# Three stages in one kernel: rounding queries and keys a step sooner, spreading GpSimd's adds, moving a column fold and a row copy

## The chip, the cores and the metric

The kernel runs on one core of one Trainium2 chip. Its time is the device time of one execution in microseconds (us), lower is better; the median of several runs is given.

## The reference, cut to what matters

All numbers are float32. Inputs of the attention are q, k, v of 4 batches x 8 heads x 576 tokens x 64.

```python
def phi(x):                                   # per head, w_phi 64 x 128
    proj = x @ w_phi
    proj = proj - max(abs(proj), axis=-1)
    return concat(exp(proj), exp(-proj))
kv = phi(k).T @ v; z = phi(k).sum(tokens)
x = (phi(q) @ kv) / (phi(q) @ z + 1e-6)       # 4 x 576 x 512 with the heads side by side
u = x + real(fft(fft(x, axis=tokens), axis=features))
un = (u - mean(u)) / sqrt(var(u) + 1e-6)
x2 = u + relu(un @ w_ch1) @ w_ch2             # hidden 2048: the first channel MLP
u2 = x2 + (relu(x2.T @ w_tok1) @ w_tok2).T    # token MLP
out = u2 + relu(u2 @ w_ch1b) @ w_ch2b         # hidden 1536: the second channel MLP
```

## The kernel before, in words

Every large product is made in three passes: each operand is rounded to a high part (ScalarE, `fp32r`), the rest is a low part (a subtraction on VectorE or GpSimd), and TensorE adds hi x hi, hi x lo and lo x hi. So each product needs a rounding and a split first.

The five engines (SP queues DMAs, TensorE, ScalarE, VectorE, GpSimd) each run one hand-written order of instructions, with waits on semaphores. An instruction that waits holds back everything behind it in its engine's order. The change touches the first stage (`front`) and its seam to the first channel MLP.

**The pair loop.** Attention goes through 16 pairs of heads, four pairs to a batch. Step k (from -1 to 15) has five sub-steps s = 0 to 4. In it TensorE projects pair k + 1 in five units (`pe_project`, L273 to L275: a rest of 64 tokens, two key units KA and KB, two query units QA and QB), turns the queries of pair k (`pe_turn`, L284, L288), makes `kv` (L302) and `num` (L316). VectorE's `dve_shift` reads each projected unit: absolute row maximum (L589), then subtraction (L597, `pm`). There are two projection banks, so a unit can be projected when the one two places before has been subtracted. ScalarE takes the exponentials (`ek` L449, `eq` L463). At s = 2 of step k VectorE normalises pair k - 1 (`dve_norm`, L602, L604, L611) into `x_all`.

**Queries and keys.** SP loads them (`load`, L220, L221) with the values (L226). ScalarE rounds them (`act_round`, L436): keys of pair k + 2 at s = 2, queries at s = 4. GpSimd splits them (`pool_split`, L716) at the start of a step: `pool_step(k)` does pair k + 2. `qk` has two buffers by parity of the pair.

**The transform.** Its symmetries halve it. For each pair's 128 columns VectorE adds the two token halves (`dve_sum`, L622, into `fold_s`) and GpSimd subtracts them (`pool_fold`, L728, into `fold_d`). Behind the third and fourth pair of a batch the columns are folded too: `dve_even` (L628) on `fold_s`, and L735 to L738 on `fold_d` and `edge`. ScalarE rounds the folded tables (`act_fold`, L483), VectorE takes the low parts (`dve_low`, L635). TensorE then does 11 pieces per batch (`pe_piece`: five "s" pieces over tokens, L322 to L325, then a cosine and a sine piece for each of three row tiles), two banks in turn. ScalarE copies (L493, L498, L501) and VectorE subtracts (`ab_lo` L644; `less`, `more` L652, L653). The pieces of batch b run one to a sub-step in steps 4b + 5 to 4b + 7. GpSimd adds the results into `x_all` (`pool_add`, four instructions L747 to L751 for each of three row tiles) and finishes token 288 (`pool_row`, L757, L758), which needs `row288`, a copy that ScalarE takes before the first add (`act_row`, L473) into one buffer, free when the row of the batch before is done (`row_done`).

The order of GpSimd's step before:

```python
        if k == PAIRS - 1:
            mlp1["gpsimd"](pool, (), 0, 2)
        for n in ready(k):
            pool_fold(pool, Pair(n))
        if k % 4 == 3 and b >= 0:
            pool_add(pool, b, 0)
            if k < PAIRS - 1:
                pool_add(pool, b, 1)
        if k % 4 == 0 and b >= 1:
            pool_add(pool, b - 1, 2)
            pool_row(pool, b - 1)
```

**The seam.** The 11 pieces of the last batch (`LAST` = 3) run inside the first block of the first channel MLP. That block has 16 hidden chunks j: `pe_first` (L983 to L985, chunk j + 2) and `pe_second` (L997 to L999, chunk j) take turns. `tensor_beside`, `scalar_beside` and `vector_beside` insert the transform's work after a chunk. ScalarE rounds the weights of a chunk (`act_weights`, L1172), GpSimd splits them (L945); `pe_first` of chunk j waits for split j + 1. At step 15 VectorE also does the normalisation of block 0 (`early_norm`: L1064 to L1071, four small steps of 1/sqrt, then L1078 three times), behind which TensorE turns the normed rows (L968). In ScalarE's order `act_row` of the last batch stands behind chunk 0 and ahead of the activation of chunk 1 (L1029); it waits for `row_done` of batch 2. GpSimd does weight chunks 2 and 3 ahead of the last two adds and the row of batch 2.

The three stages behind (first channel MLP from its second block on, token MLP, second channel MLP) are not touched.

## Time and profile before

| what | value |
|---|---|
| median of 3 runs | 1038.95 us (1037.57 to 1039.57) |
| the profiled execution | 1037.23 us, its span 1035.4 us |
| TensorE busy (PE) | 1011.9 us, 98% of the span, 7731 instructions |
| weight loads (PEld) | 905.3 us, 87% |
| VectorE / ScalarE / GpSimd busy | 391.8 us (38%) / 290.4 us (28%) / 188.1 us (18%) |
| chain that ended last | PE 91%; DVE 4%; POOL 3%; ACT 1%; issue 1% |
| mean granted TensorE clock | 0.992 of full |
| L436 rounding of queries or keys (ScalarE) | 32, median 0.67 us |
| L716 their split (GpSimd) | 32, mean 1.44 us |
| L589, L597 on VectorE | 0.69 us each for a full unit, 0.42 for the rest |
| ScalarE waits for turned queries (L463 <- L288) | 43.6 us in 22 waits |
| loads of queries or keys, issue to landing | 4.0 us median, 288 KB each |

Busy times are shares of the span from the first to the last instruction. A matmul's end is modelled, so a busy TensorE is not one at its peak. The front takes about the first 257 us; from there on TensorE hardly waits. PE, DVE, ACT, POOL and SP are TensorE, VectorE, ScalarE, GpSimd and the DMA queue of the Sync engine. In a timeline row the first number is the start, the second the duration, both in us; a bracket gives the idle time of the engine ahead of it and what ended it. The granted clock is given as a share of 2.4 GHz.

### The profile page before, as it was taken

The numbers are of one execution on the slowest core, as the hardware profiler recorded it, in microseconds if no ns is written. First come the engines' busy times: TensorE is split into PE (matmuls) and PEld (weight loads), VectorE is DVE, ScalarE is ACT, GpSimd is POOL, SyncE is SP. The second block draws the span as 40 slices with busy tenths as digits, with TensorE's granted clock in tenths as the row PEclk, the third lists the DMA queues.
The fourth block names the chain that finished last, engine by engine and source line by source line (L and its number), as shares of the span: only waits on it lengthen the run. The fifth ranks groups of instructions, "written<-read, shape, count | busy, mean of one in ns | idle before, by whom it ended". The sixth has DMA issues, their size and how long they took to land.

```text
span 1035.4 us, 18136 instructions
## 1 busy us (share of the span) xinstructions
PE 1011.9 (98%) x7731; PEld 905.3 (87%) x7731; DVE 391.8 (38%) x690; ACT 290.4 (28%) x580; POOL 188.1 (18%) x159
## 2 busy tenths in 40 slices
PE   7999999997999999999999999999999999999998
PEld 5999898986999999999999999777889899999997
DVE  5697878882142231222222213545121212121211
ACT  5765555652331111111111113243111111111110
POOL 2552735474930000000000000053100000000000
PEclk9999999998999999999999999999999999999999
DMA  5322232332601001010010120576101010101000
GB/s 174 97 81 66 73 119 73 132 134 66 191 18 62 1 31 31 1 61 0 0 61 0 48 52 1 168 242 225 46 1 61 1 62 1 61 0 61 0 32 30
DMA packets 47649, 66.34 MB, mean 64 GB/s; under 512 B 22432, under 2 KB 23392, under 8 KB 47456
## 3 DMA queue, kind: packets, MB, share of 16 engines
q1 hardware_dynamic: 45856, 59.10, 18.2%
q10 hardware_dynamic: 1728, 6.29, 1.7%
q8 instruction: 51, 0.84, 0.3%
q14 instruction: 14, 0.11, 0.0%
HBM read 46.51 MB, written 18.87 MB: 63 GB/s over the span
## 4 chain that ended last, share of the span: by engine, by line
PE 91%; DVE 4%; POOL 3%; ACT 1%; issue 1%; DMA 0%; SPq 0%; DVEq 0%; ACTq 0%; POOLq 0%
PE mlp_y L998 11%; PE mlp_y L999 11%; PE mlp_hid L985 11%; PE mlp_hid L983 11%; PE mlp_hid L984 11%; PE mlp_y L997 11%; PE num L316 3%; PE kv L302 3%; PE proj L273 2%; PE four L322 1%; PE proj L274 1%; PE proj L275 1%; PE mlp_turn_in L968 1%; PE four L325 1%; PE tok_y L1262 1%; PE four L324 1%
## 5 line engine op out<-in xcount | busy, mean ns | idle before, releaser
L1097 DVE SCALAR_TENSOR_TENSOR mlp_h_lo<-mlp_hid,mlp_h_hi 128x384 fp32r<-128x384 f32 x168 | 93.7, 558 | 468.6 <-ACT mlp_h_hi L1029 468.6
L983 PE MATMUL mlp_hid<-mlp_ut_hi,mlp_w_hi 128*128 128x384 f32 x672 | 229.2, 341 | 0.0
L985 PE MATMUL mlp_hid<-mlp_ut_hi,mlp_w_lo 128*128 128x384 f32 x672 | 226.5, 337 | 0.0
L984 PE MATMUL mlp_hid<-mlp_ut_lo,mlp_w_hi 128*128 128x384 f32 x672 | 225.5, 336 | 0.0
L1029 ACT ACTIVATE mlp_h_hi<-mlp_hid 128x384 fp32r<-128x384 f32 x168 | 82.6, 492 | 501.1 <-PE mlp_hid L985 501.1
L999 PE MATMUL mlp_y<-mlp_w_hi,mlp_h_lo 128*128 128x512 f32 x504 | 199.6, 396 | 0.0
L998 PE MATMUL mlp_y<-mlp_w_lo,mlp_h_hi 128*128 128x512 f32 x504 | 199.1, 395 | 0.0
L997 PE MATMUL mlp_y<-mlp_w_hi,mlp_h_hi 128*128 128x512 f32 x504 | 197.6, 392 | 0.4 <-DVE mlp_h_lo L1097 0.2
L945 POOL TENSOR_TENSOR mlp_w_lo<-mlp_w_raw,mlp_w_hi 128x1024 fp32r<-128x1024 f32 x26 | 62.5, 2421 | 409.8 <-DVE tok_x_lo L1317 396.5
L983 PEld LDWEIGHTS mlp_hid<-mlp_ut_hi,mlp_w_hi 128*128 128x128 f32 x672 | 126.3, 188 | 5.7 <-DVE mlp_ut_lo L1083 0.2
L984 PEld LDWEIGHTS mlp_hid<-mlp_ut_lo,mlp_w_hi 128*128 128x128 f32 x672 | 126.3, 188 | 5.3
L985 PEld LDWEIGHTS mlp_hid<-mlp_ut_hi,mlp_w_lo 128*128 128x128 f32 x672 | 126.0, 188 | 0.0
L999 PEld LDWEIGHTS mlp_y<-mlp_w_hi,mlp_h_lo 128*128 128x128 f32 x504 | 94.6, 188 | 20.4
L997 PEld LDWEIGHTS mlp_y<-mlp_w_hi,mlp_h_hi 128*128 128x128 f32 x504 | 95.0, 188 | 16.0 <-issue 0.5
L998 PEld LDWEIGHTS mlp_y<-mlp_w_lo,mlp_h_hi 128*128 128x128 f32 x504 | 94.8, 188 | 16.0
L589 DVE TENSOR_REDUCE absmax<-proj 128x4 f32<-128x512 f32 (+1 forms) x80 | 50.5, 632 | 35.3 <-PE proj L275 35.1
L716 POOL TENSOR_TENSOR qk_lo<-qk,qk_hi 128x576 fp32r<-128x576 f32 x32 | 46.1, 1444 | 96.6 <-ACT qk_hi L436 96.6
L273 PE MATMUL proj<-wphi_hi,qk_hi 128*128 128x256 f32 x144 | 48.7, 338 | 10.1 <-DVE pm L597 6.2
L463 ACT ACTIVATE eq<-pt 128x512 f32<-128x512 f32 (+1 forms) x96 | 42.0, 490 | 50.1 <-PE pt L288 43.6
L597 DVE TENSOR_TENSOR pm<-proj,absmax 128x512 f32<-128x512 f32 (+1 forms) x80 | 51.1, 638 | 5.1 <-ACT ek L449 0.5
L1083 DVE TENSOR_TENSOR mlp_ut_lo<-mlp_turn_in,mlp_ut_hi 128x384 fp32r<-128x384 f32 x44 | 24.5, 558 | 73.6 <-ACT mlp_ut_hi L1022 73.4
L449 ACT ACTIVATE ek<-pm 128x512 f32<-128x512 f32 (+1 forms) x96 | 48.4, 558 | 4.4 <-DVE pm L597 4.4
(123 smaller groups left out, 1166.4 us busy)
## 6 DMA issues: line engine op xcount, KB each, us to landing
mlp_u<-u_scratch SPq DMA_DIRECT2D x12, 768.0 KB, 4.6
mlp_w_raw<-in_w_mlp SPq DMA_DIRECT2D x14, 512.0 KB, 4.4
mlp_w_raw<-in_w_mlp ACTq DMA_DIRECT2D x12, 512.0 KB, 7.1
v<-in_v SPq DMA_DIRECT2D x16, 320.0 KB, 3.7
qk<-in_kT SPq DMA_DIRECT2D x16, 288.0 KB, 4.0
qk<-in_qT SPq DMA_DIRECT2D x16, 288.0 KB, 4.0
u_scratch<-x_all SPq DMA_DIRECT2D x4, 1152.0 KB, 6.6
x_scratch<-mlp_u SPq DMA_DIRECT2D x5, 768.0 KB, 3.6
```

Of the source, the lines that this page charges most:

```text
L273: nc.tensor.matmul(out, hi, wphi_hi[:, :], start=True, stop=False)
L589: nc.vector.tensor_reduce(absmax[:, unit, 0:cols], src, AX.X, ALU.max, apply_absolute_value=True).then_inc(absmax_done, 1)
L597: nc.vector.tensor_tensor(pm[p.parity][:, unit, 0:cols, :], src, top, ALU.subtract).then_inc(shifted, 1)
L945: nc.gpsimd.tensor_tensor(w_lo[:, nf - 1 - j, :], raw(j), w_hi[:, j, :], ALU.subtract).then_inc(w_split, 1)
L983: nc.tensor.matmul(out, w_hi[:, j, col], hi, start=(c == 0), stop=False)
L984: nc.tensor.matmul(out, w_hi[:, j, col], lo, start=False, stop=False)
L985: last = nc.tensor.matmul(out, w_lo[:, nf - 1 - j, col], hi, start=False, stop=(c == DC - 1))
L997: nc.tensor.matmul(y[t][:, :], hi, w_hi[:, j, D:2 * D], start=(j == 0), stop=False)
L998: nc.tensor.matmul(y[t][:, :], hi, w_lo[:, nf - 1 - j, D:2 * D], start=False, stop=False)
L999: last = nc.tensor.matmul(y[t][:, :], lo, w_hi[:, j, D:2 * D], start=False, stop=(j == nf - 1))
L1029: nc.scalar.activation(h_hi[:, j % 2, :], hid[j % 2][:, 0:BT], ACT.Relu).then_inc(h_rounded, 1)
L1097: nc.vector.scalar_tensor_tensor(out=h_lo[:, j % 2, :], in0=hid[j % 2][:, 0:BT], scalar=0.0, in1=h_hi[:, j % 2, :], op0=ALU.max, op1=ALU.s ...
```

## The change

Four things are moved; no arithmetic is added or left out.

- Queries and keys of pair k + 3 are both rounded at s = 4 of step k (before: keys of pair k + 2 at s = 2, queries at s = 4). `load` is split into `load_qk` and `load_v`, and the queries and keys of pair n + 1 are loaded ahead of the values of pair n. `pool_split` stays at its place.
- `pool_add` 0, 1 and 2 of a batch stand at the start of three steps (k % 4 = 3, 0, 1), ahead of `pool_fold`; `pool_row` follows the third. `pool_fold` waits for VectorE's sum of the pair, not for its normalisation.
- `dve_even` moves from s = 2 to the end of s = 4 of its step, behind the last two shifts.
- At the seam all five "s" pieces of the last batch stand behind chunk 0, the six others behind chunk 1. ScalarE's `act_row` moves behind the five pieces and behind the activation of chunk 1, and its folds come ahead of weight chunk 2. GpSimd does the last two adds and the row of batch 2 ahead of weight chunks 2 and 3. SP stores batch 2 before it loads weight chunk 6.

```diff
@@ -214,11 +214,13 @@
         return four[(len(PIECES) * b + i) % 2]
 
 
-    def load(sp, p):
+    def load_qk(sp, p):
         if p.n >= 2:
             sp.wait_ge(qk_split, 2 * p.n - 2)
         sp.dma_start(qk[:, p.parity, KEY], dram["kT"][p.n]).then_inc(k_loaded[p.parity], 16)
         sp.dma_start(qk[:, p.parity, QUERY], dram["qT"][p.n]).then_inc(q_loaded[p.parity], 16)
+
+    def load_v(sp, p):
         if p.n >= 2:
             sp.wait_ge(kv_done, p.n - 1)
         else:
@@ -233,11 +235,16 @@
     def sync(sp):
         sp.dma_start(wphi[:, :], dram["wphi"]).then_inc(consts_loaded, 16)
         sp.dma_start(ident_a[:, :], dram["ident"]).then_inc(consts_loaded, 16)
-        load(sp, Pair(0))
-        load(sp, Pair(1))
+        load_qk(sp, Pair(0))
+        load_v(sp, Pair(0))
+        load_qk(sp, Pair(1))
+        load_v(sp, Pair(1))
         sp.dma_start(table[:, 0:TCOLS], dram["table"]).then_inc(table_loaded, 16)
+        load_qk(sp, Pair(2))
         for n in range(2, PAIRS):
-            load(sp, Pair(n))
+            if n + 1 < PAIRS:
+                load_qk(sp, Pair(n + 1))
+            load_v(sp, Pair(n))
             if n in (11, 15):
                 store(sp, n // 4 - 2)
         sp.wait_ge(qk_split, 2 * PAIRS)
@@ -250,9 +257,9 @@
         mlp1["load_weights"](sp, 0, [2, 3])
         sp.wait_ge(x_done, PAIRS)
         mlp1["load_block"](sp, 1)
-        mlp1["load_weights"](sp, 4, [0, 1, 2])
+        mlp1["load_weights"](sp, 4, [0, 1])
         store(sp, 2)
-        mlp1["load_weights"](sp, 4, [3])
+        mlp1["load_weights"](sp, 4, [2, 3])
         mlp1["load_weights"](sp, 8, [0, 1, 2])
         store(sp, 3)
         mlp1["load_weights"](sp, 8, [3])
@@ -425,7 +432,7 @@
 
     def tensor_beside(pe, what, j):
 
-        for i in {("second", 0): (0, 1), ("first", 2): (2, 3), ("second", 1): range(4, len(PIECES))}.get((what, j), ()):
+        for i in {("second", 0): range(5), ("second", 1): range(5, len(PIECES))}.get((what, j), ()):
             pe_piece(pe, LAST, i)
 
 
@@ -517,8 +524,8 @@
                     act_qexp(act, p, 1)
                 if following < PAIRS:
                     act_kexp(act, Pair(following), KA)
-                if k + 2 < PAIRS:
-                    act_round(act, Pair(k + 2), KEY)
+                if k < 0:
+                    act_round(act, Pair(1), KEY)
             if s == 3:
                 if k >= 0:
                     act_kv(act, p)
@@ -526,8 +533,11 @@
                 if following < PAIRS:
                     act_kexp(act, Pair(following), KB)
             if s == 4:
-                if k + 2 < PAIRS:
-                    act_round(act, Pair(k + 2), QUERY)
+                if k < 0:
+                    act_round(act, Pair(1), QUERY)
+                if k + 3 < PAIRS:
+                    act_round(act, Pair(k + 3), KEY)
+                    act_round(act, Pair(k + 3), QUERY)
                 if k % 4 == 1 and 5 <= k:
                     act_fold(act, k // 4 - 1, 1)
                 if k % 4 == 2 and 6 <= k:
@@ -561,18 +571,17 @@
     def scalar_beside(act, j):
 
         if j == 0:
-            mlp1["act_weights"](act, [2])
             act_fold(act, LAST, 0)
             act_fold(act, LAST, 1)
-            mlp1["act_weights"](act, [3])
+            mlp1["act_weights"](act, [2, 3])
+        if j == 1:
+            for i in range(5):
+                act_piece(act, LAST, i)
             act_row(act, LAST)
-        if j == 1:
-            act_piece(act, LAST, 0)
-            act_piece(act, LAST, 1)
             act.wait_ge(fold_split, 2 * B)
             mlp1["act_weights"](act, [4])
         if j == 2:
-            for i in range(2, len(PIECES)):
+            for i in range(5, len(PIECES)):
                 act_piece(act, LAST, i)
             mlp1["act_weights"](act, [5])
         if j == 3:
@@ -665,8 +674,8 @@
                 dve_norm(dve, Pair(k - 1))
                 for n in [0, 1, 2] if k == 3 else [k - 1] if k > 3 else []:
                     dve_sum(dve, Pair(n))
-                    if n % 4 >= 2:
-                        dve_even(dve, n // 4, n % 4 - 2)
+            if s == 4 and k >= 3 and (k - 1) % 4 >= 2:
+                dve_even(dve, (k - 1) // 4, (k - 1) % 4 - 2)
             if s == 4 and k % 4 == 1 and 5 <= k:
                 dve_low(dve, k // 4 - 1, 1)
             if s == 4 and k == PAIRS - 2:
@@ -700,10 +709,10 @@
             dve_low(dve, LAST, 0)
             dve_low(dve, LAST, 1)
         if j == 1:
-            dve_piece(dve, LAST, 0)
-            dve_piece(dve, LAST, 1)
+            for i in range(5):
+                dve_piece(dve, LAST, i)
         if j == 2:
-            for i in range(2, len(PIECES)):
+            for i in range(5, len(PIECES)):
                 dve_piece(dve, LAST, i)
         if j == 9:
             dve.wait_ge(row_done, B)
@@ -719,7 +728,7 @@
     def pool_fold(pool, p):
         b, i = p.n // 4, p.n % 4
         cols = slice(2 * DH * i, 2 * DH * i + 2 * DH)
-        pool.wait_ge(x_done, p.n + 1)
+        pool.wait_ge(summed, p.n + 1)
         if b > 0:
             pool.wait_ge(fold_split, 2 * b)
         else:
@@ -765,27 +774,27 @@
             pool.wait_ge(table_rounded, k + 1)
             nc.gpsimd.tensor_tensor(table_lo[:, THIRD[k]], table[:, THIRD[k]], table_hi[:, THIRD[k]],
                                     ALU.subtract).then_inc(table_split, 1)
+        if k % 4 == 3 and b >= 0:
+            pool_add(pool, b, 0)
+        if k % 4 == 0 and b >= 1:
+            pool_add(pool, b - 1, 1)
+        if k % 4 == 1 and b >= 1:
+            pool_add(pool, b - 1, 2)
+            pool_row(pool, b - 1)
         if k == PAIRS - 1:
             mlp1["gpsimd"](pool, (), 0, 2)
         for n in ready(k):
             pool_fold(pool, Pair(n))
-        if k % 4 == 3 and b >= 0:
-            pool_add(pool, b, 0)
-            if k < PAIRS - 1:
-                pool_add(pool, b, 1)
-        if k % 4 == 0 and b >= 1:
-            pool_add(pool, b - 1, 2)
-            pool_row(pool, b - 1)
 
     def gpsimd(pool):
         pool_split(pool, Pair(0))
         for k in range(-1, PAIRS):
             pool_step(pool, k)
         pool_fold(pool, Pair(PAIRS - 1))
-        mlp1["gpsimd"](pool, (), 2, 4)
         pool_add(pool, LAST - 1, 1)
         pool_add(pool, LAST - 1, 2)
         pool_row(pool, LAST - 1)
+        mlp1["gpsimd"](pool, (), 2, 4)
         pool_add(pool, LAST, 0)
         pool.wait_ge(d_done, 2 * FRONT * B)
         mlp1["gpsimd"](pool, (), 4, 6)
```

## Rows read from the trace of the kernel before

**Rows 1.** TensorE's waits, whole span: us in total, times, longest us.
```profile
PE four L322 <- DVE ab_lo L644: 6.8, 1, 6.8
...
PE proj L273 <- DVE pm L597: 6.2, 8, 2.2
```

**Rows 2.** Busy time by stretch: PE, PEld, DVE, ACT, POOL, clock, DMA, GB/s.
```profile
120.00:130.00 10.00, 7.77 (x133) 7.25 (x131) 8.81 (x11) 4.00 (x9) 9.71 (x13) 0.83 0.30 87
...
240.00:250.00 10.00, 7.47 (x30) 5.96 (x31) 2.75 (x6) 3.69 (x8) 0.43 (x1) 0.58 0.59 170
```

**Rows 3.** TensorE's timeline, num products of a pair: start us, us, what.
```profile
67.00 3.02 PE L316 MATMUL num<-kvs,eq 128*64 128x65 f32 x96
...
78.52 3.02 PE L316 MATMUL num<-kvs,eq 128*64 128x65 f32 x96
...
119.80 3.02 PE L316 MATMUL num<-kvs,eq 128*64 128x65 f32 x96
...
135.07 3.02 PE L316 MATMUL num<-kvs,eq 128*64 128x65 f32 x96
...
176.33 3.02 PE L316 MATMUL num<-kvs,eq 128*64 128x65 f32 x96
...
190.55 3.02 PE L316 MATMUL num<-kvs,eq 128*64 128x65 f32 x96
...
218.89 3.02 PE L316 MATMUL num<-kvs,eq 128*64 128x65 f32 x96
```

**Rows 4.** Timeline 117 to 123.5 us, VectorE and GpSimd.
```profile
118.43 2.09 DVE L622 TENSOR_TENSOR table<-x_all 96x384 f32<-96x384 f32 x1
...
120.56 3.03 DVE L628 TENSOR_TENSOR table<-table 96x384 f32<-96x384 f32 x1
...
119.48 0.62 POOL L751 TENSOR_TENSOR x_all<-x_all,less 96x255 f32<-96x255 f32 x1
...
120.07 3.10 POOL L716 TENSOR_TENSOR qk_lo<-qk,qk_hi 128x576 fp32r<-128x576 f32 x2
```

**Rows 5.** Source line L628: duration ns min/median/max, first, last start.
```profile
L628 DVE TENSOR_TENSOR table<-table x8: 551/1776/3029, 57.2 to 225.1; 96x381 f32<-96x381 f32 x4, 96x384 f32<-96x384 f32 x4
```

**Rows 6.** Timeline around 111 us, VectorE and GpSimd.
```profile
110.83 0.41 DVE L653 TENSOR_TENSOR more<-even,four 96x258 f32<-96x258 f32 x1
...
110.99 1.41 POOL L716 TENSOR_TENSOR qk_lo<-qk,qk_hi 128x576 fp32r<-128x576 f32 x1 [3.46 <-ACT qk_hi L436]
```

**Rows 7.** Timeline around 211 us and 294 us, VectorE and GpSimd.
```profile
211.00 0.41 DVE L653 TENSOR_TENSOR more<-even,four 96x258 f32<-96x258 f32 x1
...
211.53 0.16 DVE L1066 TENSOR_TENSOR mlp_step<-mlp_rstd 128x3 f32<-128x3 f32 x1
...
211.73 0.16 DVE L1068 SCALAR_TENSOR_TENSOR mlp_step<-mlp_step,mlp_var_eps 128x3 f32<-128x3 f32 x1
...
294.17 2.38 POOL L945 TENSOR_TENSOR mlp_w_lo<-mlp_w_raw,mlp_w_hi 128x1024 fp32r<-128x1024 f32 x1 [1.80 <-ACT mlp_w_hi L1172]
...
294.26 2.32 DVE L1071 SCALAR_TENSOR_TENSOR mlp_rstd<-mlp_step,mlp_rstd 128x3 f32<-128x3 f32 x1
```

**Rows 8.** Timeline 223 to 259 us, VectorE, GpSimd, ScalarE, TensorE.
```profile
223.99 0.74 DVE L622 TENSOR_TENSOR table<-x_all 96x384 f32<-96x384 f32 x1
...
228.35 5.54 DVE L635 TENSOR_TENSOR fold_lo<-table,fold_hi 97x774 fp32r<-97x774 f32 x2 [1.19 <-ACT fold_hi L483]
...
227.59 5.48 POOL L945 TENSOR_TENSOR mlp_w_lo<-mlp_w_raw,mlp_w_hi 128x1024 fp32r<-128x1024 f32 x2
...
240.52 0.62 ACT L473 COPY row<-x_all 1x512 f32<-1x512 f32 x1 [10.59 <-POOL x_all L758]
...
249.66 0.30 PE L322 MATMUL four<-table_hi,fold_hi 96*128 96x288 f32 x1
...
256.88 0.34 PE L983 MATMUL mlp_hid<-mlp_ut_hi,mlp_w_hi 128*128 128x384 f32 x1
...
258.96 0.39 PE L997 MATMUL mlp_y<-mlp_w_hi,mlp_h_hi 128*128 128x512 f32 x1
```

## The prediction

> **What bounds the kernel now.** I read the page first: TensorE is busy 98% of the span (first line of the table above), so time can only be gained where it stands still, runs at the lower clock, or waits inside matmuls. The list of waits names two such places: 6.8 us once, before a product of the transform, released by VectorE's low part, and 6.2 us in 8 pieces before projections, released by the subtraction of the row maximum (pm) [rows 1]. The table of stretches adds the clock: 0.83 in 120 to 130 us, 0.58 in 240 to 250 us [rows 2]. I then took TensorE's timeline and used the start of the 96 "num" products as a clock for the pair loop [rows 3]. From pair 4 to pair 5 it takes 78.52 - 67.00 = 11.52 us with no wait in it. The same work takes 135.07 - 119.80 = 15.27 us from pair 8 to 9 and 190.55 - 176.33 = 14.22 us from pair 12 to 13. So 3.75 and 2.70 us are lost there. Both have the same wait of 2.2 us; only the first falls to the lower clock, so a fall costs about 1.05 us. Behind pair 3 there is a small loss of the same kind.
>
> Who makes VectorE late there: the row sum (L622) takes 2.09 us and the column fold (L628) 3.03 us [rows 4], against 0.55 us at best for the fold, and for the sum of the same size [rows 5]. GpSimd is working through four adds and two splits just then. The fold ends 0.5 us after the second split. VectorE's operation with two operands in SBUF stands until GpSimd's run ends. It is let in between the last add and the split (118.43 + 2.09 = 120.52, GpSimd's add ended 120.10), but not between the four adds, nor between the two splits.
>
> The large wait is at the end: ScalarE waits 10.59 us to copy row 288 of the last batch [rows 8], because GpSimd does two weight chunks before the adds and the row of batch 2. Everything behind the copy in ScalarE's order, then VectorE, then TensorE, is late.
>
> **The change, part by part.**
>
> (1) *Pairs 8 and 12.* GpSimd's adds are spread and `pool_fold` waits for the row sum, so GpSimd is idle when that sum comes: 0.55 us in place of 2.09. The fold leaves its place ahead of the last two key and query shifts. Together they take 5.1 - 0.55 = 4.6 us out from in front of a wait of 2.2 us. What is late next is the fold itself, which now stands ahead of the next pair's first shift. It is requested about 121.75 (sum done at 119.0, then two shifts of two operations of 0.69), while GpSimd is in the last instruction of its fold; then come two splits. Let in at that border, it costs nothing and the whole 3.75 and 2.70 come back. If it is let in only behind both splits (two of 1.4 us), TensorE waits 1.9 us. I take 3.75 and 2.70, as the border add to split is of this kind; lower ends 1.9 and 0.8.
>
> (2) *Pairs 7 and 11.* The fold of batch 1 (and 2) used to hide ahead of shifts that were early. It now follows VectorE's "more", which ends at 111.24 and can come up to 0.4 us earlier, while GpSimd starts its split at 110.99 [rows 6]. If VectorE is first, nothing is lost; if not, it waits for both splits (2.8 us) and the next first shift, for which I estimate 1.6 us of room in TensorE's timeline, comes 1.2 us late. I take 0.4 each, ends 0 and 1.2. *Pair 3:* three sums now compete with three GpSimd folds that start behind each sum; gain 0.4 to loss 1.1, taken as 0.
>
> (3) *Queries and keys a step sooner.* 32 roundings and 32 splits stay, as do all DMAs. No pair but the first two was late by them, so I cost the move at nothing. Cover: ScalarE waits 43.6 us in 22 waits for the turned queries, most of it right behind the new place, and both roundings are 1.3 us (table above). On SP the loads of pair n + 1 stand ahead of the values of pair n; both are needed a step later and a load lands in 4.0 us. If that cover were gone, each pair would pay the 1.3 us. On ScalarE the second rounding of `fold_hi` comes 0.65 us later at pairs 5, 9, 13, where GpSimd is no longer in VectorE's way: 0.
>
> (4) *Pair 15: a new collision.* The first add of batch 2 now comes ahead of the weight chunks, and is released by the same "more" (211.00 + 0.41) that VectorE follows with the four small steps of 1/sqrt (0.2 us apart, [rows 7]). These have operands in SBUF. That such a tiny one is blocked is shown further on: L1071 took 2.32 us and ended with GpSimd's 2.38 us chunk [rows 7]. So L1068 waits for the four adds (to about 214.4), L1071 for the first weight chunk (to 216.9), and the normed rows, 213.6 before, come at 218.6. Behind them on VectorE are "less/more", the normalisation of pair 14 and its row sum. The normalisation ends at 220.8, and the num products of pair 15, which started at 218.89 [rows 3], wait for it: 1.95 us lost. If GpSimd is also ahead of L1066, which starts 0.12 us after "more", one turn more is lost: 4.5 us. The two starts are too close to tell; I take the middle, 3.3.
>
> The Trainium skill, "SBUF — State Buffer", section "SBUF: two separate sides", says that the port pair of GpSimd and VectorE is locked for one whole instruction and then given up. By that rule L1068 would wait for one add of 0.7 us only and this part would cost nothing. The trace shows 2.09 us behind four adds, so I do not follow it here.
>
> (5) *The end of the front.* Count from the start of num 15 (before 218.89) to the fourth hidden chunk (before 256.88): 38.0 us [rows 3, 8]. Now ScalarE's copy stands behind five pieces, and GpSimd does adds and row before chunks 2 and 3. The bound becomes GpSimd. Row sum 15 ended 5.8 us behind num 15 (223.99 + 0.74), and with the column fold of batch 2 now ahead of it comes at 6.3. GpSimd's fold takes 3.3 us, with VectorE's last column fold let in, 3.85; then one low part of VectorE (0.9), an add of 2.75 (four instructions of 0.6 to 0.7), the other low part (0.9), an add (2.75), the row (two of 0.7) and weight chunk 2 (2.4). Sum 21.25. Then TensorE: chunk 2, 2.1 (258.96 - 256.88), its y product 2.1, and six pieces, 6.1 (seven took 256.88 - 249.66 = 7.2). Sum 31.55, gain 6.5. If VectorE's low part is not let in ahead of the first add, 2.8 less: 3.7. (The low parts: two in 5.54 us, of which about 3.7 are waits for the chunks.) If chunk 2 is not what TensorE waits for, its own work and the two conversions give 8.3. Two stalls of about 2 us remain, each of a size at which the clock fell once and once not: 1.05 each at risk, taken as 0.
>
> Sum: 3.75 + 2.70 - 0.8 - 3.3 + 6.5 = 8.9 us. The profiled execution took 1037.23 us (span 1035.4); less 8.9 is 1028.3. The median of the runs is 1.7 above the profiled one, so I forecast **1030.0 us**.
>
> **The rivals.**
>
> *A. VectorE is let in at every instruction of GpSimd.* Then (2) and (4) cost nothing: 3.75 + 2.7 + 6.5 = 13 us, 1026.0. This is the skill's rule above ("SBUF — State Buffer"). For it: the low part L635 got in between the two weight chunks [rows 8]. Against: the four adds and the pair of splits [rows 4]. Chance 0.15.
>
> *B. Late turns eat half.* The folds are let in only behind the splits (pairs 8, 12: 2.7 us returned in place of 6.45; pairs 7, 11: 1.2 lost each) and the rest as in the sum: 2.7 - 2.4 - 3.3 + 6.5 = 3.5 us, 1035.5. For it: the fold's 3.03 us went past the border of two splits. Against: it needs GpSimd to win four near races. Chance 0.22.
>
> *C. Slower: the 1/sqrt chain at pair 15.* It loses three turns (4.5 us) and its late normalisation puts the last sum, fold and low parts of batch 3 behind GpSimd's adds, so that the tail gives only 3.7; with the clock fallen at the waits (two of 1.05) and B's turns lost (2.7 - 2.4): 0.3 - 4.5 + 3.7 - 2.1 = -2.6, so 1041.6. It decides once the chain ends after about 219. For it: the collision is certain, only its length is open. Against: all turns must be lost. Chance 0.07.
>
> *D. No difference.* B with three turns lost in the chain: 3.5 - 1.2 - 1.05 (clock) = 1.2 us, 1037.7. Chance 0.08.
>
> **How the numbers follow.** The forecast, with its own range of 1027 to 1033.5, has 0.48; A 0.15, B 0.22, D 0.08, C 0.07. The range leaves out C, D and the far half of A: 1025.5 to 1036.8. About 0.2% (2.1 us) is what a measurement of this kernel can tell from no change. Faster 0.84 (forecast, A, nearly all of B), same 0.09, slower 0.07.
>
> **What the profile of the changed kernel would show.** (1) right: num 8 to 9 and num 12 to 13 take 11.5 to 12 us, L622 there 0.55; wrong if 13 or more. (2): L628 at pairs 7 and 11 takes 0.55 (VectorE first) or 3 us. (4) right: L1068 and L1071 take 2 to 3 us each, and num 13 to num 15 takes 30.3 to 32.8 us in place of 218.89 - 190.55 = 28.3 [rows 3]; wrong if they take 0.16. (5) right: ScalarE's wait for row 288 is gone and TensorE's longest wait in the tail is about 2 us, for the third weight chunk, after 31 to 32 us. The forecast falls if a wait for a query or key shows up on TensorE or if ScalarE's roundings stand in front of an exponential that TensorE waits for.

## The result, and the profile after

The changed kernel takes 1035.8 us (median of 20 runs, 1034.1 to 1038.4), the kernel before beside it on the same chip 1037.95 us (20 runs): ratio 0.9982, interval 0.9974 to 0.9989. That is faster by 2.15 us. 8.9 us were forecast. The time lies inside the range, at its upper end, but three quarters of the gain are missing.

The profiled execution took 1037.61 us (span 1035.8), which is 1.8 above the median of its own runs, so its span says nothing of a gain. A second profile of the same kernel took 1035.41 us (span 1033.6). I therefore read distances between fixed marks, with both profiles side by side. The first view is TensorE's timeline of the changed kernel, the starts of the num products of pairs 4, 8, 9, 12, 13, 14 and 15. They answer to [rows 3]; pair 4 and 14 are new.

```profile
72.22 3.02 PE L323 MATMUL num<-kvs,eq 128*64 128x65 f32 x96
...
124.99 3.02 PE L323 MATMUL num<-kvs,eq 128*64 128x65 f32 x96
...
137.95 3.02 PE L323 MATMUL num<-kvs,eq 128*64 128x65 f32 x96
...
179.21 3.02 PE L323 MATMUL num<-kvs,eq 128*64 128x65 f32 x96
...
192.18 3.02 PE L323 MATMUL num<-kvs,eq 128*64 128x65 f32 x96
...
208.28 3.02 PE L323 MATMUL num<-kvs,eq 128*64 128x65 f32 x96
...
223.68 4.25 PE L323 MATMUL num<-kvs,eq 128*64 128x65 f32 x96 [0.36 <-DVE x_all L620]
```

In the same view num 3 starts at 56.29. Worked out from such starts (us; "tail" is from num 15 to the fourth hidden chunk, "undisturbed" what the same step takes with nothing late; the other kernels of this study have their numbers with them):

| kernel | num 3 to 4 | 8 to 9 | 12 to 13 | 14 to 15 | tail |
|---|---|---|---|---|---|
| before | 11.18 | 15.27 | 14.22 | 12.23 | 37.99 |
| after, first profile | 15.93 | 12.96 | 12.97 | 15.40 | 33.56 |
| after, second profile | 17.18 | 12.98 | 12.98 | 15.40 | 31.15 |
| undisturbed | 11.2 | 11.5 | 11.5 | 12.2 | |

So against the kernel before the first profile has +4.75, -2.31, -1.25, +3.17 and -4.43, and the first num product starts 0.57 later (its key came later by 0.5): sum +0.5, and the span grew by 0.4. The second has +6.00, -2.29, -1.24, +3.17, -6.84 and an earlier start by 0.50: sum -1.7, and the span shrank by 1.8. No other step moved by more than about 0.1 us.

TensorE's list of waits over the whole span of the changed kernel (first profile):

```profile
PE proj L280 <- DVE pm L606: 7.5, 6, 3.8
PE proj L280 <- POOL qk_lo L725: 5.2, 2, 2.7
PE mlp_hid L992 <- POOL mlp_w_lo L954: 2.6, 1, 2.6
PE mlp_turn_in L977 <- DVE mlp_un L1087: 2.4, 1, 2.4
```

The wait of 6.8 us of [rows 1] is gone. In its place stand 2.6 us for a weight chunk and 2.4 us for the normed rows, and the wait for pm is larger than before (7.5 us against 6.2), with one piece of 3.8 us. The 5.2 us for the splits are at the start, where the loads arrive.

**Pair 3** is the largest loss, and has the piece of 3.8 us. The timeline of VectorE, GpSimd and TensorE from 55 to 67 us:

```profile
55.23 2.30 DVE L631 TENSOR_TENSOR table<-x_all 96x384 f32<-96x384 f32 x3
...
60.10 3.98 DVE L637 TENSOR_TENSOR table<-table 96x381 f32<-96x381 f32 x1
...
59.97 0.99 POOL L747 TENSOR_TENSOR table<-table 96x381 f32<-96x381 f32 x1
60.92 2.75 POOL L725 TENSOR_TENSOR qk_lo<-qk,qk_hi 128x576 fp32r<-128x576 f32 x2
...
65.00 0.39 PE L280 MATMUL proj<-wphi_hi,qk_hi 128*128 128x256 f32 x1 [3.78 <-DVE pm L606]
```

The column fold starts four VectorE operations behind the sums, when GpSimd has one instruction of its own fold and two splits in a row to do. It is let in when the second split ends (63.67) and takes 3.98 us for work of 0.55. Behind the wait the granted clock falls, from 60 to 70 us (columns as in [rows 2]; a slice's clock is its mean, and 0.83 or 0.67 is a slice in part at 2.4 GHz and in part at 1.2 GHz). In the second profile it is 0.66 there behind the same wait of 3.8 us, which goes with the difference between 15.9 and 17.2:

```profile
60.00:70.00 10.00, 6.22 (x91) 5.51 (x91) 9.22 (x12) 3.93 (x8) 4.03 (x4) 0.83 0.01 2
...
240.00:250.00 10.00, 7.41 (x29) 6.82 (x29) 1.54 (x4) 2.74 (x5) 6.23 (x5) 0.67 0.68 219
```

**Pair 8**, the same two engines at 123.6 to 130 us (the lines that answer to [rows 4]):

```profile
123.61 0.55 DVE L631 TENSOR_TENSOR table<-x_all 96x384 f32<-96x384 f32 x1
...
126.81 3.34 DVE L637 TENSOR_TENSOR table<-table 96x384 f32<-96x384 f32 x1
...
125.98 1.00 POOL L747 TENSOR_TENSOR table<-table 96x384 f32<-96x384 f32 x1
126.95 2.79 POOL L725 TENSOR_TENSOR qk_lo<-qk,qk_hi 128x576 fp32r<-128x576 f32 x2
```

The sum is down to 0.55 us as forecast, the fold is not: 3.34 us instead of 3.03, in a later place.

**Pair 15**, VectorE and GpSimd from 213 to 221 us (to be laid beside [rows 7]):

```profile
213.34 0.58 DVE L1077 SCALAR_TENSOR_TENSOR mlp_step<-mlp_step,mlp_var_eps 128x3 f32<-128x3 f32 x1
213.96 0.65 DVE L1080 SCALAR_TENSOR_TENSOR mlp_rstd<-mlp_step,mlp_rstd 128x3 f32<-128x3 f32 x1
214.65 6.90 DVE L1087 TENSOR_SCALAR mlp_un<-mlp_u,mlp_mean_var,mlp_rstd 128x512 f32<-128x512 f32 x3
...
213.17 0.73 POOL L756 TENSOR_TENSOR x_all<-x_all,less 96x257 f32<-96x257 f32 x1 [8.00 <-DVE more L662]
213.87 0.72 POOL L757 TENSOR_TENSOR x_all<-x_all,more 96x255 f32<-96x255 f32 x1
...
216.11 4.69 POOL L954 TENSOR_TENSOR mlp_w_lo<-mlp_raw_early,mlp_w_hi 128x1024 fp32r<-128x1024 f32 x2
```

The collision is there, but the small steps of 1/sqrt get in at the borders of GpSimd's adds (0.58 and 0.65 us instead of 0.16). What stands is the normalisation itself: three operations that take 1.46 us alone take 6.90 us and end with the second weight chunk. It is the second of the three that stands. The first takes 0.92 us; the second is asked for at 215.49, under the last add, and ends with the chunks (VectorE's timeline, 216 to 221 us):

```profile
215.49 5.60 DVE L1087 TENSOR_SCALAR mlp_un<-mlp_u,mlp_mean_var,mlp_rstd 128x512 f32<-128x512 f32 x1
```

**The tail**, GpSimd's row and chunk 2 and the product that waits for it (beside [rows 8]):

```profile
241.02 0.72 POOL L767 TENSOR_TENSOR x_all<-row,even 1x255 f32<-1x255 f32 x1
241.71 4.66 POOL L954 TENSOR_TENSOR mlp_w_lo<-mlp_w_raw,mlp_w_hi 128x1024 fp32r<-128x1024 f32 x2
...
244.19 0.66 PE L992 MATMUL mlp_hid<-mlp_ut_hi,mlp_w_hi 128*128 128x384 f32 x1 [2.59 <-POOL mlp_w_lo L954]
```

### The profile page after: what moved, and what is told of

Read it like the earlier page. It is cut to its first block, busy times and chain, and to the rows that moved or that the text cites. A ratio compares the mean times of both kernels' runs of the same rounds, so it can differ in the third digit from the quotient of the medians.

```text
span 1035.8 us, 18136 instructions
## 1 busy us (share of the span) xinstructions
PE 1012.5 (98%) x7731; PEld 906.9 (88%) x7731; DVE 388.8 (38%) x690; ACT 292.5 (28%) x580; POOL 188.8 (18%) x159
## 4 chain that ended last, share of the span: by engine, by line
PE 91%; DVE 5%; POOL 2%; ACT 1%; issue 1%; DMA 0%; SPq 0%; DVEq 0%; ACTq 0%; POOLq 0%
PE mlp_hid L992 11%; PE mlp_hid L994 11%; PE mlp_y L1007 11%; PE mlp_y L1008 11%; PE mlp_hid L993 11%; PE mlp_y L1006 11%; PE num L323 4%; PE kv L309 3%; PE proj L280 2%; PE four L329 1%; PE mlp_turn_in L977 1%; PE proj L282 1%; PE proj L281 1%; PE tok_y L1271 1%; PE four L332 1%; PE pt L295 1%
## 5 line engine op out<-in xcount | busy, mean ns | idle before, releaser
L1008 PEld LDWEIGHTS mlp_y<-mlp_w_hi,mlp_h_lo 128*128 128x128 f32 x504 | 94.8, 188 | 20.5
L323 PEld LDWEIGHTS num<-kvs,eq 128*64 128x64 f32 x1536 | 47.4, 140 | 2.9 <-issue 2.0
```

The lines of the kernel that those rows point to most:

```text
L323: last = nc.tensor.matmul(num[64 * half:64 * half + 64, col:col + V1], eq_flat[:, first:first + 64], kvs[:, h, V1 * sign:V1 * sign + V1], ...
L1008: last = nc.tensor.matmul(y[t][:, :], lo, w_hi[:, j, D:2 * D], start=False, stop=(j == nf - 1))
```

## The experiments

Undoing parts of the change first. My theory after the result: the late column fold costs at pairs 3, 8 and 12, the early first add costs at pair 15, and the rest is as forecast. The rival: the earlier rounding, which lets GpSimd's splits follow at once, is what crowds pair 3.

**The column fold back beside the sum** (the rest as changed):

```
                     dve_sum(dve, Pair(n))
+                    if n % 4 >= 2:
+                        dve_even(dve, n // 4, n % 4 - 2)
-            if s == 4 and k >= 3 and (k - 1) % 4 >= 2:
-                dve_even(dve, (k - 1) // 4, (k - 1) % 4 - 2)
```

> The changed kernel with the column fold (dve_even) back at s = 2, right behind the row sums. Theory (VectorE's operation on SBUF data is held by a run of GpSimd instructions, and the fold's new place puts it behind such a run): the 3.98 us fold behind pair 3 takes 0.55 us, num 3 to num 4 falls from 15.9 to about 11.2 us, num 8 to 9 and num 12 to 13 fall from 13.0 to about 11.5 us; in all 7.7 us less than the changed kernel, a ratio to the kernel before of about 0.991. Rival (the roundings and splits a step sooner crowd ScalarE and GpSimd at pair 3): num 3 to 4 stays above 15 us and the total within 2 us of the changed kernel.

Measured: 1027.58 us, ratio 0.9902 (0.9886 to 0.9917). Steps 11.77, 11.51, 11.5, 16.08 and tail 31.39. The fold's new place costs 4.2 us at pair 3 (5.4 against the second profile) and 1.45 us at each of pairs 8 and 12: 7.1 or 8.3 together, and 8.25 us lie between the medians (1035.83 less 1027.58). Pair 15 loses 0.7 us more here than in the changed kernel.

**Step 15's first add behind the two weight chunks** (the rest as changed):

```
+        if k == PAIRS - 1:
+            mlp1["gpsimd"](pool, (), 0, 2)
         if k % 4 == 3 and b >= 0:
             pool_add(pool, b, 0)
```

> The changed kernel with one order undone: at step 15 GpSimd does weight chunks 0 and 1 ahead of the first add of batch 2, as before. Theory (the three subtractions that make the normed rows, 6.90 us in place of 1.46, are held by GpSimd's adds and chunks): they take 1.5 us, num 14 to 15 falls from 15.4 to about 12.3 us, 3.1 us less in all, ratio about 0.995. Rival (the normed rows are late because the 1/sqrt or its inputs are late, or the chunks alone hold them): num 14 to 15 stays above 14 us.

Measured: 1032.61 us, ratio 0.9948 (0.9935 to 0.9961), 3.2 us less than the changed kernel. The step from num 14 to 15 is 12.24 again. The other steps are as in the second profile of the changed kernel (17.19, 12.97, 12.98, tail 31.31). The three normalisations take 1.46 us.

**Both of these:**

> The changed kernel with both undone: column fold at s = 2, and chunks 0 and 1 ahead of the first add at step 15. Theory: the two gains add, 7.7 + 3.1 = 10.8 us less than the changed kernel, about 1025 us, ratio 0.988. Rival (the time lost at one place is made up by a wait further on): less than 7 us in all.

Measured: 1023.71 us, ratio 0.9857 (0.9843 to 0.9871), steps 11.77, 11.51, 11.5, 12.23, tail 31.29. The two losses add up, to 12.1 us (8.25 and 3.2 each by itself).

**The kernel before with the earlier loading and rounding alone** (the rounding of both halves of pair k + 3 at the end of step k, and the loads in that order; adds, folds and tail as before):

> The kernel before with one part of the change alone: queries and keys loaded and rounded a step sooner. Theory: no wait of TensorE was on them, so the total stays within 1 us of the kernel before; num 3 to 4 stays about 11.2 us. Rival (crowding at pair 3): num 3 to 4 goes above 13 us and the total is 2 us or more slower.

Measured: 1035.63 us, ratio 0.9980 (0.9971 to 0.9989), 2.1 us faster where I expected no more than 1 us either way, and the near balance has another reason than the one I gave. Num 3 to 4 takes 17.12 us, so the rival's mechanism is there. Num 8 to 9 and 12 to 13 take 11.51 and 11.5, so the earlier loading and rounding by itself gives back all that was lost there. The timeline of this kernel at pair 3, VectorE and GpSimd:

```profile
54.61 3.22 DVE L632 TENSOR_TENSOR table<-x_all 96x384 f32<-96x384 f32 x3
57.86 3.94 DVE L638 TENSOR_TENSOR table<-table 96x381 f32<-96x381 f32 x1
...
53.44 3.25 POOL L738 TENSOR_TENSOR table<-x_all 96x384 f32<-96x384 f32 x3
...
57.49 1.19 POOL L748 TENSOR_TENSOR table<-table 96x381 f32<-96x381 f32 x1
58.64 2.75 POOL L726 TENSOR_TENSOR qk_lo<-qk,qk_hi 128x576 fp32r<-128x576 f32 x2
```

GpSimd used to wait for ScalarE between its fold and each split ([rows 6] shows such a wait of 3.46 us). With the rounding done, fold and splits run as one piece, and the fold of VectorE that falls into it stands to the end. At pair 8 the same thing helps: adds and splits are through (122.46 us) before the sum (124.17 us).

**The same with GpSimd's folds waiting for the sum**, as the change has it:

```
-        pool.wait_ge(x_done, p.n + 1)
+        pool.wait_ge(summed, p.n + 1)
```

> The kernel of the earlier run with queries and keys rounded a step sooner alone, and in it GpSimd's folds wait for VectorE's sum, as in the change, instead of for the scaled values. Theory: at pair 3 the earlier folds held VectorE's three sums (3.22 us) and pushed the column fold under the splits; with the wait the sums take 2.3 and the column fold 1.3 us before the splits begin, and the step from num 3 to num 4 falls from 17.1 to 11.8; pairs 8 and 12 stay at 11.5; ratio 0.992 to 0.9935. Rival: the splits that follow sooner cost pair 3 whatever the folds wait for: above 15 us, ratio 0.998.

Measured: 1030.26 us, ratio 0.9927 (0.9915 to 0.9940). Num 3 to 4 takes 11.77 us; pairs 8 and 12 take 11.77 and 11.82, the tail 37.9. This one wait is worth 5.4 us, all of it at pair 3: the sums take 2.30 us and the fold 1.25 us (at 56.88), beside GpSimd's fold and ahead of its splits (60.55).

**The changed kernel with the splits of pair 6 behind the fold of pair 3:**

```
-        if k + 2 < PAIRS:
+        if k + 2 < PAIRS and k != 4:
             pool_split(pool, Pair(k + 2))
...
             pool_fold(pool, Pair(n))
+        if k == 4:
+            pool_split(pool, Pair(k + 2))
```

> The changed kernel with GpSimd's two rounding splits of pair 6 put behind the fold of pair 3 instead of directly behind the fold of pair 2. Theory: the 3.98 us of the column fold at 60.1 us are time under those two splits: it falls to 1.2 to 2.3 (one instruction of GpSimd's fold beside it at most), the step from num 3 to num 4 from 15.9 to 11.5 to 12.5, ratio to the kernel before 0.994 to 0.995. Rival: the fold is held by GpSimd's own fold (L747) or by its place behind four reductions: it stays over 3 us and the step over 15, ratio 0.998.

Measured: 1035.32 us, ratio 0.9977 (0.9968 to 0.9986). The theory holds at its place and the time misses. The fold of pair 3's step takes 1.29 us and num 3 to 4 11.68 us, but num 4 to 5, 11.5 in the changed kernel, now takes 15.41. VectorE and GpSimd at 68 to 75 us:

```profile
69.55 5.78 DVE L637 TENSOR_TENSOR table<-table 96x384 f32<-96x384 f32 x1
...
68.44 1.00 POOL L747 TENSOR_TENSOR table<-table 96x384 f32<-96x384 f32 x1
69.40 5.52 POOL L725 TENSOR_TENSOR qk_lo<-qk,qk_hi 128x576 fp32r<-128x576 f32 x4
```

Now the next late fold meets four splits in a row and stands for all four. So it is the run of splits that holds it, wherever they meet.

**The kernel before with only the adds spread over three steps:**

> The kernel before with only GpSimd's adds spread over three steps (one each at steps 3, 4 and 5 of a batch, ahead of the step's folds; step 15 and the tail as before). Theory, since the earlier rounding alone freed pairs 8 and 12: the spreading by itself frees little there, since the splits still stand behind ScalarE's rounding and come late beside the sum: num 8 to 9 and 12 to 13 stay over 13, ratio 0.996 or above. The forecast's reason, that two adds on top of one another held the sum: both fall to 11.5, together 6.4 us less, ratio 0.994.

Measured: 1034.77 us, ratio 0.9971 (0.9961 to 0.9981). My theory of that time missed: num 8 to 9 and 12 to 13 fall to 11.53 each, and the sum takes 0.55 us. The forecast's reason was right. Earlier rounding and spreading each give the whole 6.45 us, and the two together give it once. The time is not the 6.4 us lower because num 9 to 10 takes 18.03 instead of 16.11 us (TensorE's wait "PE num L316 <- ACT kvs L468", 1.9 us; its cause is shown with the last kernel below) and there are smaller losses behind it (15.20 for 14.85, 13.16 for 12.23, tail 38.7).

**The kernel before with only the tail's part of the change:**

> The kernel before with only the change's parts of the tail (adds and row ahead of chunks 2 and 3 on GpSimd, pieces five and four, row 288's copy behind the first five pieces, the queue's order). Theory: the tail's part stands by itself: distances up to num 15 as before (15.3, 14.2 and 12.2 at pairs 8, 12 and 15), num 15 to chunk 3 falls from 38.0 to 33.6 or, with full clock, 31.3; ratio 0.9935 to 0.9960. Rival: the tail's gain needs the adds that were done earlier in the steps: above 36, ratio above 0.998.

Measured: 1030.98 us, ratio 0.9939 (0.9925 to 0.9952). Tail 31.10, steps as before (15.44, 14.22, 12.23). The tail's part is independent of the others and worth 6.9 us.

**The changed kernel once more:**

> The changed kernel itself once more, for a second profile of it. Theory: what differs between its runs is the clock behind the 2.6 us wait for chunk 2 (0.67 in the slice 240 to 250 in its first profile, 1.00 in the kernel that differs from it only at pair 4): pairs 3, 8, 12 and 15 repeat within 0.3 us (15.9, 13.0, 13.0, 15.4), the wait of 2.6 us repeats, and the distance from num 15 to chunk 3 lies anywhere between 30 and 34. Rival: the tail repeats at 33.6, and the other kernel's 30.1 comes from its different order at pair 4.

Measured: 1035.83 us, ratio 0.9984 (0.9973 to 0.9995). Pairs 8, 12 and 15 repeat within 0.02 us and so does the wait for chunk 2 (2.60), while the tail is 31.15. Pair 3 did not repeat (17.18 against 15.93). Both differences go with the clock: the slice 240 to 250 us has 0.83 here and 0.67 in the first profile, the slice 220 to 230 us, in which num 15 runs, 1.00 and 0.83, the slice 60 to 70 us 0.66 and 0.83. In the kernel with the moved splits the tail was 30.11 at a clock of 1.00 (240 to 250 us) with the same wait. From the product that waited (243.39, 243.21 and 244.19 us) to the fourth hidden chunk it is 10.25, 11.82 and 13.05 us of the same work in the three profiles, so the clock behind the same wait makes up to 2.8 us.

**Chunk 2 between the adds**, on top of both moves undone:

```
         pool_add(pool, LAST - 1, 1)
+        mlp1["gpsimd"](pool, (), 2, 3)
         pool_add(pool, LAST - 1, 2)
         pool_row(pool, LAST - 1)
-        mlp1["gpsimd"](pool, (), 2, 4)
+        mlp1["gpsimd"](pool, (), 3, 4)
```

> The kernel with both moves undone (column fold back beside the sum, step 15's first add behind the two weight chunks), and weight chunk 2's split put between GpSimd's add 1 and add 2 of the third batch. Theory: TensorE's wait of 2.6 us for chunk 2's low half, and the slow clock behind it, are what is left of the tail's loss: the wait goes, the low half lands 2.9 us sooner, the slice 230 to 240 is at full clock, the distance from num 15 to chunk 3 falls from 31.3 to 28 or less, ratio to the kernel before 0.982 to 0.984. Rival: the adds and the row that are now later hold ScalarE and TensorE's rounds of the last fold: the wait moves there and the distance stays at 31, ratio 0.986 to 0.988.

Measured: 1020.29 us (1019.3 to 1021.5), ratio 0.9836 (0.9823 to 0.9850): the fastest kernel of this study, 15.5 us under the changed one and 17.6 under the kernel before. Tail 26.95, 4.3 us less than with chunk 2 behind the row: the 2.6 us of waiting and the low clock behind them. GpSimd's lines and the clock of this kernel:

```profile
224.07 0.64 POOL L760 TENSOR_TENSOR x_all<-x_all,less 96x255 f32<-96x255 f32 x1
224.67 2.39 POOL L955 TENSOR_TENSOR mlp_w_lo<-mlp_w_raw,mlp_w_hi 128x1024 fp32r<-128x1024 f32 x1
227.03 0.73 POOL L756 TENSOR_TENSOR x_all<-x_all,less 96x257 f32<-96x257 f32 x1
...
230.68 0.73 POOL L767 TENSOR_TENSOR x_all<-row,even 1x255 f32<-1x255 f32 x1
```

```profile
230.00:240.00 10.00, 10.00 (x64) 8.61 (x63) 2.82 (x7) 4.39 (x8) 7.37 (x8) 1.00 0.71 218
```

The adds that are now later hold nobody.

**Is the earlier rounding needed?** Spreading, tail and chunk 2 between the adds on the kernel before; the loads, the rounding and the folds' wait as they were:

> The kernel before with the spreading of the adds, the tail's parts and chunk 2 between the adds, but the rounding where it was, the column fold beside the sum and step 15's first add behind chunks and fold as before: all that the best kernel has except the earlier rounding and the folds' wait for the sum. Theory: spreading alone frees pairs 8 and 12, but once they are on time ScalarE's rounding of a key half stands ahead of its copy of the key-value product and holds TensorE's numerator by 1.9 us at pair 9 (18.0 instead of 16.1, as in the run with spreading alone); so 2 to 5 us slower than with the earlier rounding, ratio 0.986 to 0.989. Rival: that wait is an accident of one run and the earlier rounding is worth nothing: pair 9 at 16.1, ratio 0.983 to 0.984.

Measured: 1024.22 us, ratio 0.9869 (0.9855 to 0.9883), 3.9 us more than in the fastest kernel. Num 9 to 10 takes 18.08 us again, with the wait of 1.9 us for the copy of the key-value product. ScalarE, TensorE and the DMA queue at that place:

```profile
139.59 0.35 SPq L231 DMA_DIRECT2D u_scratch<-x_all  x1
139.99 0.50 SPq L220 DMA_DIRECT2D qk<-in_kT  x1
...
147.93 0.67 ACT L436 CAST qk_hi<-qk 128x576 fp32r<-128x576 f32 x1 [4.72 <-DMA qk<-in_kT]
...
148.80 0.38 ACT L468 COPY kvs<-kv 128x260 f32<-128x260 f32 x1
...
149.62 4.60 PE L316 MATMUL num<-kvs,eq 128*64 128x65 f32 x96 [1.91 <-ACT kvs L468]
```

The rounding of pair 12's keys stands in ScalarE's order in front of the copy that the num products wait for, as I expected. But a rounding takes 0.67 us only, and what makes it late is something I had not looked for: its keys have not landed. SP stores batch 0 before it loads them. The row of that batch is done a step later when the adds are spread, and SP waits 10.4 us for it. So the store starts at 139.59 us, where it started at 132.80 in the kernel before, and the keys are issued right behind it, at 139.99 (133.53 in the kernel before); ScalarE can round them 7.9 us later. With spreading alone it is the same: the store at 140.66, ScalarE's wait for the keys 4.7 us. In the kernel before ScalarE does not wait for keys there. In the changed kernel these keys are loaded ahead of that store. So here the change's order of loads can be what helps as well as its place of the rounding; no run has one without the other, and this kernel also lacks the folds' wait for the sum. The next step takes 16.44 us instead of 14.85 because the clock has fallen behind the wait: num 10 takes 4.60 us instead of 3.02 (slice 150 to 160 us: 0.83).

## Why the prediction was wrong, point by point

- **(3), "No pair but the first two was late by them, so I cost the move at nothing", and (2), "Pair 3 ... taken as 0": these steps failed, and with them most of the sum.** I asked only who waits for the roundings, and not what GpSimd does once its splits no longer wait. The move alone is worth 3.76 and 2.7 us at pairs 8 and 12 and costs 5.9 us at pair 3 (the kernel with earlier rounding alone). In the change, pair 3 costs 4.75 and 6.0 us in the two profiles, where I allowed 1.1 at most. There the loss hangs on the column fold's new place, which I followed at pairs 8 and 12 but not at pair 3: with the fold back beside the sum, the step takes 11.77 us against 11.18 before, with the splits moved from behind it 11.68. What the late fold would cost at pair 3 without the earlier rounding, no run shows. The price I named, 1.3 us for each pair, was for a cover on ScalarE and DMA that did hold. The folds' wait for the sum, which I used only at pairs 8 and 12, is what would have cured pair 3 (17.12 to 11.77), had the column fold stayed beside the sum. Nor is the move worth nothing elsewhere: without it the spread adds make pair 12's keys late behind the store of batch 0 (1.9 us of waiting, in two kernels).
- **(1), "Let in at that border, it costs nothing and the whole 3.75 and 2.70 come back": failed.** The fold came just when I worked out (1.82 us behind num 8's start, against 1.95), with GpSimd in the last instruction of its fold, and was let in only behind both splits: 3.34 us. 2.3 and 1.25 us came back, 3.55 instead of 6.45. The lower ends (1.9 and 0.8) were nearer, and this is what rival B said of pairs 8 and 12. That the sum falls to 0.55 us was right. The reason for the gain was right too (spreading alone gives 3.74 and 2.69), but half the change does it already, and the late fold only takes from it.
- **(2), pairs 7 and 11, 0.4 each:** VectorE was first both times (L637 0.55 us at 116.07 and 170.30), so nothing was lost.
- **(4), 3.3 us: the size was right, the mechanism not.** The loss is 3.17 us in both profiles, and putting the add back gives 3.2. But L1077 and L1080 took 0.58 and 0.65 us, where I had 2 to 3 each; the normalisation behind them, which I had left out as free, took 5.4 us more than alone, so that the size came out right by luck. The Trainium skill's rule ("SBUF — State Buffer", section "SBUF: two separate sides"), by which the operation that starts first has the pair for its whole instruction, fits the two small steps and the first normalisation (0.92 us), each let in behind one add, and fails for the second, which stood across the border of the last add and that between the two chunks (5.60 us). The measurements decide for neither in general.
- **(5), 6.5 us: right.** The chain of GpSimd gave chunk 2's low half 20.5 and 19.3 us behind num 15 (21.25 forecast), the longest wait there is TensorE's for that chunk (2.6), ScalarE's wait for row 288 is gone, and the tail fell to 31.15 (31.5 forecast). In the first profile it fell to 33.56 only: num 15 itself took 4.25 us there instead of 3.02 (slice 220 to 230 us at a clock of 0.83; 1.00 in the second profile), and behind the wait the work forecast at 10.3 us took 13.05 at a clock of 0.67 (11.82 in the second profile). I had named that risk at 1.05 us and taken it as 0; it was worth 1.5 and 2.8.
- **The sum by what was measured** (second profile): 3.53 + 0 - 6.00 - 3.17 + 6.84 = 1.2 us, and 0.5 for the earlier start, against 1.8 in the spans and 2.15 in the medians. The gap of 7.7 to the forecast of 8.9 is pair 3 (6.0) and pairs 8 and 12 (2.9), less what pairs 7 and 11 did not cost (0.8), what pair 15 cost less (0.1) and what the tail gave more (0.3).
- Rivals: A (each border lets VectorE in) fell with three folds of 3.3 to 4.0 us (pairs 3, 8 and 12). B came near in time (1035.5), by its losses at pairs 8 and 12, but without those at 7 and 11 and with pair 3, which it did not have: the time fell into the stated range by luck, and also because the forecast started from a median of 1038.95, 1.0 us above the kernel before as it was measured beside the changed one. C's and D's chains of lost turns did not occur.

**What stays open** is which border between two GpSimd instructions lets VectorE in. It got in between GpSimd's adds at pair 15, and between two chunks in [rows 8]; it was kept out between splits (2 and 4 of them in a row), between a fold and a split, between the last add and the chunks and between the two chunks at pair 15, and between four adds in [rows 4]. No run here separates length, operands or the time at which VectorE asks. Nor was it tried how much of the move in (3) is the order of the loads and how much the place of the rounding, or why the same wait lowers the clock by different amounts from run to run.

## What to carry to other kernels

When work is moved earlier, ask what its consumer does once it needn't wait: an engine that used to pause between its pieces now runs them as one block, and an operation of another engine that it keeps out can stand for the whole block. When work is moved later, ask what is queued behind it: here a store waited for the later row, and a load that was needed sooner stood behind the store. Put VectorE's operation with two SBUF operands where the other engine surely waits (here, right behind the sum that GpSimd waits for), not where it has "room". Cost every part of a change by itself and the pairs of them too: of four parts here one gave 6.9 us, two each gave the same 6.45 us at pairs 8 and 12, and two places undid most of it; with those undone and one more chunk moved, the kernel is 1.6% faster instead of 0.2%.

## What the runs showed of the hardware that I had not expected

- A VectorE operation can stand across four GpSimd instructions (5.78 us beside four splits of 1.4 us), and in the same run another, of 0.16 us by itself, is let in after one add (0.59 us).
- An operation that has one tensor operand in SBUF and two columns of scalars (L1087, 128x512, 0.54 us by itself) is held just like one with two tensors: one of the three took 5.60 us.
- The same wait of TensorE, 2.6 us, was followed by a granted clock between 0.67 and 1.00 in the slice around it, in kernels that are the same from there on, and the work behind it took 10.25 to 13.05 us. Whether this makes the spread between runs is not shown: the changed kernel's 20 runs spread over 4.3 us and the 5 of the kernel without the wait over 2.2 us, but the 5 of the kernel with step 15's add behind the chunks, which has the same wait, over 0.7 us.
